# A folded weight product in quarters, four load buffers for the attention steps, and weights loaded in the stage that uses them

## The reference, cut to what matters

```python
def reference(q, k, v, w1, w2, w3, w_out, u1, u2, u3, uo):
    # q, k, v: 8 batches x 8 heads x 576 x 64; D[h][i][j] = gamma_h ** (i - j) for i >= j, else 0
    x = ((q @ k.T) / 8 * D) @ v                    # to 4608 tokens x 512
    x = max(x @ w1, x @ w2, x @ w3) @ w_out        # 512 -> 768 -> 512
    return ((x @ u1) * (x @ u2)) @ u3 @ uo         # 512 -> 1024 -> 1024 -> 512
```

## Time and profile before

| | |
|---|---|
| Time, median of 3 runs | 1333.28 us (1332.85 to 1336.16) |
| The profiled execution | 1333.16 us, of which the span 1331.4 us |
| TensorE busy | 1259.7 us (95%) |
| VectorE, ScalarE, POOL busy | 803.4, 459.7, 452.3 us |
| DMA | 174.37 MB, mean 131 GB/s |

### The profile page before, as it was taken

How to read it: one execution, slowest core, us unless ns; L and a number is a source line. 1 busy time by engine, 2 the same in 40 slices (tenths; PEclk the granted TensorE clock), 3 DMA queues, 4 the chain that set the end, 5 groups by cost and what they waited for, 6 DMA issues and landing times.

```text
span 1331.4 us, 20535 instructions
## 1 busy us (share of the span) xinstructions
PE 1259.7 (95%) x8032; PEld 1235.0 (93%) x8032; DVE 803.4 (60%) x1194; ACT 459.7 (35%) x707; POOL 452.3 (34%) x248
## 2 busy tenths in 40 slices
PE   6999878999999999999999999999999998499999
PEld 5888867999999999999899999999999997499999
DVE  5555668656455555548889677454535537756762
ACT  2112112433333232325455444232323323344442
POOL 2333566602020202006598562202012007635550
PEclk8999988999999999999999999999999999799999
DMA  8778786302020202031655541313313133334441
GB/s 312 235 239 288 252 286 223 133 29 95 25 95 31 89 31 90 31 137 54 224 180 176 174 157 53 109 48 101 104 58 102 52 130 120 130 137 148 155 142 66
DMA packets 82929, 174.37 MB, mean 131 GB/s; under 512 B 8976, under 2 KB 57488, under 8 KB 82832
## 3 DMA queue, kind: packets, MB, share of 16 engines
q1 hardware_dynamic: 82832, 173.05, 37.9%
HBM read 109.58 MB, written 63.44 MB: 130 GB/s over the span
## 4 chain that ended last, share of the span: by engine, by line
PE 74%; DMA 10%; DVE 9%; issue 4%; POOL 1%; SPq 1%; ACT 1%; DVEq 0%; POOLq 0%
PE ps L944 23%; PE ps L945 23%; PE ps L946 23%; DVE clo L699 3%; DMA vks<-vk 3%; DMA u3raw<-u3T 2%; DVE wlo L699 2%; DMA x2d<-h 2%; DMA gd<-h 1%; PE ps L890 1%; PE ps L875 1%; PE ps L900 1%; DVE state L728 1%; DVE probs L709 1%; POOL qdec L499 1%
## 5 line engine op out<-in xcount | busy, mean ns | idle before, releaser
L944 PE MATMUL ps<-chi,whi 128*128 128x384 f32 x2016 | 678.7, 337 | 32.4 <-DVE wlo L699 15.3
L945 PE MATMUL ps<-clo,whi 128*128 128x384 f32 x2016 | 676.4, 336 | 0.0
L946 PE MATMUL ps<-chi,wlo 128*128 128x384 f32 x2016 | 676.3, 335 | 0.0
L499 POOL TENSOR_TENSOR raw<-raw,raw 128x768 f32<-128x768 f32 (+2 forms) x96 | 273.3, 2866 | 536.7 <-DMA raw<-xd 222.0
L944 PEld LDWEIGHTS ps<-chi,whi 128*128 128x128 f32 x2016 | 380.7, 189 | 37.9 <-issue 18.6
L945 PEld LDWEIGHTS ps<-clo,whi 128*128 128x128 f32 x2016 | 380.9, 189 | 0.0
L946 PEld LDWEIGHTS ps<-chi,wlo 128*128 128x128 f32 x2016 | 380.7, 189 | 0.0
L699 DVE TENSOR_TENSOR clo<-raw,chi 128x768 fp32r<-128x768 f32 (+2 forms) x168 | 259.5, 1567 | 16.5 <-ACT chi L622 16.1
L622 ACT CAST chi<-raw 128x768 fp32r<-128x768 f32 (+2 forms) x168 | 180.7, 1081 | 93.8 <-PE ps L946 86.6
L689 ACT COPY w<-ps 128x384 f32<-128x384 f32 x126 | 60.8, 482 | 253.7 <-PE ps L946 252.2
L675 ACT COPY u<-ps 128x384 f32<-128x384 f32 x126 | 60.8, 482 | 168.1 <-PE ps L946 166.6
(11 more groups left out here) (41 smaller groups left out, 917.1 us busy)
## 6 DMA issues: line engine op xcount, KB each, us to landing
qks<-qk SPq DMA_DIRECT2D x32, 576.0 KB, 4.4
vks<-vk SPq DMA_DIRECT2D x32, 576.0 KB, 6.0
gd<-h SPq DMA_DIRECT2D x96, 192.0 KB, 1.9
raw<-gd SPq DMA_DIRECT2D x24, 768.0 KB, 7.2
hd<-h SPq DMA_DIRECT2D x72, 192.0 KB, 1.9
raw<-hd SPq DMA_DIRECT2D x24, 576.0 KB, 5.7
raw<-xd SPq DMA_DIRECT2D x24, 384.0 KB, 5.4
x2d<-h SPq DMA_DIRECT2D x48, 192.0 KB, 2.5
```

Of the source, the lines that this page charges most:

```text
L499: return nc.gpsimd.tensor_tensor(out_, a, b, op)
L944: nc.tensor.matmul(to, w1, x1, start=(start and k == 0), stop=False, skip_group_check=True)
L945: nc.tensor.matmul(to, w1, x2, start=False, stop=False, skip_group_check=True)
L946: last = nc.tensor.matmul(to, w2, x1, start=False, stop=(k == KH[st] - 1), skip_group_check=True)
```

## The change

The 8 blocks of the folded product are cut into quarters (6 matmuls each, over two of the eight slices). Step n does quarter n - 2, for n from 2 to 31, and step 32, which has no scores, does the last two. Loads, casts, splits and copies of `u3`, `uo` and the product follow that rhythm: `u3` block kb is loaded at step 4 kb - 2, cast at 4 kb, split at 4 kb + 1.

`qks` gets 4 buffers instead of 2, `vks` 4 instead of 3, both loaded three steps ahead; `qdec` gets 2. `vks` now lies where positions 4 to 6 of the first token tile are kept, so these are cast and split in the first iterations of stage B, once `valued` is complete. VectorE does a step's splits before `make_state` instead of behind it.

Only weights 0 and 1 and the first tile's raw tokens are loaded in the steps (steps 8, 10 and 12). Weights 2 to 8 are loaded from iteration 0 of stage B on, and each is cast and split in the iteration in which it is summed, one earlier than before.

```diff
 def due(std, ci, io, it, point):
     out = []
-    for tau in range(1, 4 * TILES):
+    for tau in range(4 * TILES):
         table = ci if tau == I * TILES else io if tau == O * TILES else std
-        if it == last_of(tau - 1):
+        if tau and it == last_of(tau - 1):
...
         if it == first_of(tau):
-            out += [(tau, pos) for pos in table.get(("next", point), [])]
+            out += [(tau, pos) for pos in table.get(("next", point), []) if tau or pos > 3]
...
-W_LOAD_AT = {6: 0, 7: 1, 8: 2, 9: 49,
+W_LOAD_AT = {2: 0, 3: 0, 4: 0, 5: 1, 6: 2, 7: 3, 8: 4, 9: 49,
...
-W_SUM_AT = {5: 0, 6: 1, 7: 2, 8: 3, 9: 50,
+W_SUM_AT = {2: 0, 3: 1, 4: 2, 5: 3, 6: 4, 7: 5, 8: 6, 9: 50,
...
-W_SPLIT_AT = {wi: it + 1 for wi, it in W_SUM_AT.items()}
+W_SPLIT_AT = {wi: it + (wi >= FIRST_W[C]) for wi, it in W_SUM_AT.items()}
...
-WC_AT = {3 + 2 * kb: kb for kb in range(FT2)}
 STEPS = NP + 1
-P1_W_LOAD = {12: 0, 14: 1, 19: 2, 20: 3, 21: 4, 23: 5}
...
+WC_FROM = 2
+QUARTERS = 4 * FT2
+def quarters(n):
+    if n == NP:
+        return range(NP - WC_FROM, QUARTERS)
+    return range(n - WC_FROM, n - WC_FROM + 1) if n >= WC_FROM else ()
+U3_LOAD = {max(4 * kb - 2, 0): kb for kb in range(1, FT2)}
+U3_HI = {max(4 * kb, 1): kb for kb in range(FT2)}
+U3_LO = {max(4 * kb + 1, 1): kb for kb in range(FT2)}
+UO_AT = {1: 0, 2: 1, 3: 2, 4: 3}
+WC_READ = {4 * kb + 3 + WC_FROM: kb for kb in range(FT2 - 1)}
+P1_W_LOAD = {8: 0, 10: 1}
+P1_W_SUM = {10: 0, 12: 1}
+P1_RAW = 12
...
         def _(sp):
             def load_qk(n):
-                if n >= 2:
-                    sp.wait_ge(scored, n - 1)
-                    sp.wait_ge(q_decayed, n - 1)
+                if n >= 4:
+                    sp.wait_ge(scored, n - 3)
+                    sp.wait_ge(q_decayed, n - 3)
...
             def load_vk(n):
-                if n >= 3:
-                    sp.wait_ge(valued, n - 2)
+                if n >= 4:
+                    sp.wait_ge(valued, n - 3)
...
-                if 2 <= wi <= 5:
+                if 2 <= wi <= 8:
+                    sp.wait_ge(valued, NP)
                     sp.wait_ge(wc_done, FT2)
+                if wi == 5:
                     for i in range(2):
                         sp.wait_ge(wc_stored[i], 32 * FT2 // 2)
...
             load_qk(0)
             sp.dma_start(dec[:, :, :], decay).then_inc(dec_loaded, 16)
+            load_vk(0)
             sp.dma_start(vtab[:, :, :], vdecay).then_inc(vtab_loaded, 16)
-            load_vk(0)
             sp.dma_start(qtab[:, :, :], qdecay).then_inc(qtab_loaded, 16)
             load_qk(1)
             load_vk(1)
+            load_u3(0)
+            load_uo(0)
+            load_qk(2)
             load_vk(2)
-            load_u3(0)
...
+            load_uo(1)
             for n in range(STEPS):
-                if n + 2 < NP:
-                    load_qk(n + 2)
...
+                if n + 3 < NP:
+                    load_qk(n + 3)
+                if n in U3_LOAD:
+                    load_u3(U3_LOAD[n])
...
+                if n + 3 < NP:
+                    load_vk(n + 3)
                 if n >= 1:
-                    if n + 2 < NP:
-                        load_vk(n + 2)
                     store_x(n - 1)
+                if n - 1 in WC_READ:
+                    store_wc(WC_READ[n - 1])
+            store_wc(FT2 - 1)
...
             def decay_queries(n):
...
-                else:
-                    pool.wait_ge(queried, n)
+                if n >= 2:
+                    pool.wait_ge(queried, n - 1)
...
         def _(act):
             for n in range(STEPS):
+                if n in U3_HI:
+                    split_u3(U3_HI[n])
+                if n in UO_AT:
+                    split_uo(UO_AT[n])
+                if n in WC_READ:
+                    read_wc(WC_READ[n])
                 if n >= 1:
                     read_values(n - 1)
...
+            read_wc(FT2 - 1)
...
         def _(dve):
             for n in range(STEPS):
                 if n < NP:
                     decay_scores(n)
-                    make_state(n)
+                if n in U3_LO:
+                    split_u3(U3_LO[n])
+                if n in UO_AT:
+                    split_uo(UO_AT[n])
...
+                if n < NP:
+                    make_state(n)
...
         def _(pe):
+            def wc_quarter(i):
+                kb, part = divmod(i, 4)
+                if part == 0:
+                    pe.wait_ge(u3_lo, kb + 1)
+                    if kb:
+                        pe.wait_ge(wc_out, kb)
+                if kb == 0:
+                    pe.wait_ge(uo_lo, part + 1)
+                to = ps[:, S_WC, :]
+                for k in (2 * part, 2 * part + 1):
...
             for n in range(STEPS):
                 if n < NP:
                     scores(n)
-                if n in WC_AT:
-                    wc_block(WC_AT[n])
+                for i in quarters(n):
+                    wc_quarter(i)
                 if n >= 1:
                     query_state(n - 1)
```

More of the change, by code:

```diff
@@ L240, in build @@
         wcst = at("wcst", [P, 2, 4, P], f32, o); o += 4096
[L241 to L247, removed]
+        qks = [at(f"qks{i}", [P, KQ_COLS], f32, o + i * KQ_COLS * 4) for i in range(4)]
+        o += 4 * KQ_COLS * 4
+        vks = [at(f"vks{i}", [P, VK_COLS], f32, comb_base[B] + 4 * 6144 + i * VK_COLS * 4) for i in range(4)]
         probs = at("probs", [P, 2, 2, SEQ], f32, o); o += 4 * SEQ * 4
@@ L252, in build @@
         vdec = at("vdec", [P, NC, P], f32, o); o += NC * P * 4
-        qdec = at("qdec", [P, NC, CH], f32, o); o += NC * CH * 4
+        qdec = [at(f"qdec{i}", [P, NC, CH], f32, o + i * NC * CH * 4) for i in range(2)]
+        o += 2 * NC * CH * 4
         state = at("state", [P, NC, P], f32, o); o += NC * P * 4
@@ L459, in _ @@
             for it in range(G + 1):
-                for wi in range(6, NW):
+                for wi in range(2, NW):
                     if W_LOAD_AT.get(wi) == it:
@@ L615, in split_tokens @@
                 if tau == 0:
[L616 to L617 removed]
+                    if pos > 3:
+                        act.wait_ge(valued, NP)
                 elif tau % TILES == 0:
@@ L678, in _ @@
                 splits(it, "p2")
-                for wi in range(5, NW):
+                for wi in range(2, NW):
                     if W_SPLIT_AT.get(wi) == it:
@@ L859, in scores @@
                         keys = SEQ + c * CH
-                        nc.tensor.matmul(ps[:, h, c * CH:(c + 1) * CH], qks[own, n % 2, keys:keys + CH],
-                                         qks[own, n % 2, c * CH:(c + 1) * CH],
+                        nc.tensor.matmul(ps[:, h, c * CH:(c + 1) * CH], qks[n % 4][own, keys:keys + CH],
+                                         qks[n % 4][own, c * CH:(c + 1) * CH],
                                          start=(c == 0), stop=(c == NC - 1), skip_group_check=True)
@@ L864, in scores @@
                     own = slice(h * DH, h * DH + DH)
-                    last = nc.tensor.matmul(ps[:, S_TAIL[h], 0:TAIL], qks[own, n % 2, KQ_COLS - CH:KQ_COLS],
-                                            qks[own, n % 2, SEQ - TAIL:SEQ],
+                    last = nc.tensor.matmul(ps[:, S_TAIL[h], 0:TAIL], qks[n % 4][own, KQ_COLS - CH:KQ_COLS],
+                                            qks[n % 4][own, SEQ - TAIL:SEQ],
                                             start=True, stop=True, skip_group_check=True)
@@ L889, in query_state @@
                     bank, cols = x_cols(c)
-                    last = nc.tensor.matmul(ps[:, bank, cols], state[:, c - 1, :], qdec[:, c - 1, 0:min(CH, SEQ - c * CH)],
+                    last = nc.tensor.matmul(ps[:, bank, cols], state[:, c - 1, :], qdec[n % 2][:, c - 1, 0:min(CH, SEQ - c * CH)],
                                             start=(c == 1 or c == NC), stop=False, skip_group_check=True)
@@ L899, in values @@
                         own = slice(h * DH, h * DH + DH)
-                        last = nc.tensor.matmul(ps[own, bank, cols], vks[n % 3][:, c * P + h * DH:c * P + h * DH + DH],
+                        last = nc.tensor.matmul(ps[own, bank, cols], vks[n % 4][:, c * P + h * DH:c * P + h * DH + DH],
                                                 probs[:, n % 2, h, c * CH:min(SEQ, (c + 1) * CH)],
@@ L903, in values @@
                 last.then_inc(valued, 1)
-            def wc_block(kb):
-                pe.wait_ge(u3_lo, kb + 1)
-                if kb:
-                    pe.wait_ge(wc_out, kb)
-                for k in range(FT2):
-                    if kb == 0 and k % 2 == 0:
-                        pe.wait_ge(uo_lo, k // 2 + 1)
-                    nc.tensor.matmul(ps[:, S_WC, :], u3hi[kb % 2][:, k, :], uohi[:, k, :], start=(k == 0), stop=False)
-                    nc.tensor.matmul(ps[:, S_WC, :], u3hi[kb % 2][:, k, :], uolo[:, k, :], start=False, stop=False)
-                    last = nc.tensor.matmul(ps[:, S_WC, :], u3lo[kb % 2][:, k, :], uohi[:, k, :],
```

(12 more changed lines are left out.)

78 lines of the change are left out of this document (26 added, 52 removed).

## The result

| | before | after |
|---|---|---|
| Median | 1334.72 us (4 runs) | 1297.39 us (4 runs) |
| Ratio after to before | | 0.9718 (95% interval 0.9697 to 0.9739) |
| Profiled execution, its span | 1333.16, 1331.4 | 1297.43, 1295.7 |
| First product of stage B starts at | 235.53 | 197.67 |
| From there to the end of the span | 1095.9 | 1098.0 |

What follows compares the result with a forecast made beforehand. TensorE was taken as the bound, with 51.5 us lost to lateness in the attention stage. Terms: 40.8 - (1.4 - 0.6) - 2.6 - 2 = 35.4 us off 1333.16, so 1298 us, range 1291 to 1311.

Steps and rivals of the forecast that it cites:

- (a): Attention steps: with quarters each takes 5.75 us instead of 9.85 and 4.38 in turn; TensorE's 184.0 us stay.
- (b): Attention loads: issued up to three steps ahead, they cause waits costed at zero after step 2.
- (c): Attention transfers: 1.67 MB per step take 5.0 us at 332 GB/s, under 5.75; cost 0, bound above 10 us.
- (d): Start and attention total: step 2 starts at 17.2, attention ends at 194.7 against 235.53; gain 40.8 us.
- (e): Joint with stage B: TensorE waits 1.4 us for wc_out, and 0.61 us of waiting at the s copy is saved.
- (f): Stage B's first unit: weight 2, loaded only then, delays s(1) and perhaps w(0); loss 2 to 3 us, taken as 2.6.
- (g): VectorE crowded by splits beside POOL: 1 us in stage B's first tile, 1 us in steps 10 to 23.
- the rival in which transfers bind: Attention stage: at 290 GB/s +10, 1308 us, chance 0.08; at 260 GB/s 1330 us, no change, chance 0.02.
- Rival 1: Attention steps: VectorE's splits before make_state make TensorE wait for the state, +10 us, 1308; chance 0.09.

Runs made afterwards that it cites:

- e2_shallow: Changed kernel with queries/keys and values/keys loaded two steps ahead instead of three; 1305.8 us.
- e6_traffic: Changed kernel with one more transfer, 0.59 MB DRAM to DRAM read by nobody, in each of steps 4 to 29; 1298.9 us.
- e1: Changed kernel with its deeper loads, but the folded product in whole blocks in every second step from 5 to 19; 1300.9 us.
- e3: Changed kernel with make_state ahead of the step's splits on VectorE, as before the change; 1317.1 us.
- e4_joint: Changed kernel with ScalarE's last copy of the folded product ahead of its last copy of x; 1297.4 us.
- e8: Changed kernel with whole product blocks and loads two steps ahead together, qdec's second buffer kept; 1305.4 us.
- e5: e4_joint with loads of weights 2, 3 and 4 issued once the folded product is done, ahead of the last stores; 1294.1 us.
- e10_split_early: Changed kernel with make_state ahead of the splits and VectorE's split of a u3 block one step earlier; 1310.2 us.

## Why the prediction was right, and where it was not

- **(a), (b) right in effect.** Steps of 5.77 us (forecast 5.75), no vdec wait after step 2. That the third step of lead is needed only at two places was not seen, nor that POOL's 45.2 us behind the loads say little: in e2_shallow it waited 78.4.
- **(c) wrong in size.** "In a stretch with the engines 0.98 busy they moved 332 GB/s" was taken for their limit. 407 GB/s were moved in e6_traffic with no step longer. TensorE was the bound by a wide margin, not a small one, and the rival in which transfers bind had little in its favour.
- **(d) close.** Step 2 started at 18.00 instead of 17.2, and the last attention matmul ended at 196.3 instead of 194.7, 1.6 us. Half of that is the start: the first step's values decay began 0.4 us later, behind vtab, and step 1 took 5.76 us where it took 5.32 (its first 16 matmuls 2.08 instead of 1.77). The rest is 29 steps at 0.02 us more and a last step 0.2 longer.
- **(e) half right.** The wait was 1.38 (forecast 1.4). The 0.6 us to be saved at the s copy were not: TensorE still waited 0.57 there. ScalarE was idle when the product was done (its copy runs from 199.01 to 199.49, after 1.55 us of idling), so this wait is the copy itself, and was so in the earlier trace rows too.
- **(f) and the clock against each other.** The first unit took 2.44 us more than before (forecast 2.6), but not for the forecast reason alone. The wait for s(1) was 0.73, not 2.6, because TensorE got there later, at half the clock from 200 to 203. Without that, e1 to e3 show it at 1.5, and the first unit still 1.6 us longer than before. So (f) took about 1 us too much, and the granted clock gave it back; the first half's cast fitted before w(0) here, though not in e4_joint, where TensorE came earlier and waited 0.85 us.
- **(g) wrong.** "1 us for them, and 1 us for the same crowding": behind the first unit, stage B kept its distance to the kernel before (counted from its first product, 2.44 us later after unit 0, 2.26 after unit 5, 2.2 at the end), and no attention step was longer for its splits. That VectorE and POOL slow each other down is in the trace (POOL's first sum of weight 2 took 1.50 us beside VectorE's clo, and the four sums of a weight 3.7 to 4.6 us, not the 2.9 of (f)), but on engines with time to spare.
- **The sum was lucky.** The gain on the profiled execution was 35.7 us, the forecast 35.4. In it (d) promised 1.6 us too much and (e) 0.6, and (g) took off 2 us that did not come; the errors cancel.
- **Rival 1** had the danger in the wrong place. I asked what splits ahead of make_state would cost; they cost nothing, and behind it they would have cost 19.7 us.
- **What the sum could not say.** It rested on TensorE's own work being the floor, and in the steps it was right because every cause of lateness was removed at once: TensorE was busy 176.00 of 176 us. It says nothing on which part carried the gain, and its tale of deeper loads and even steps was too simple. By the runs, undoing quarters and depth together costs 8.0 us; on top of that weights 2 to 4 in the steps cost 6.8, late tokens 6.6, and tight due dates of u3 with make_state first 5.3. That is 26.7 of 37.3, if they add, which was not run; quarters and depth did not (3.5 and 8.4 alone, 8.0 together), and the last three sizes are good to a few us only. What is left, some 10 us, was not tried by itself: the rest of the start (step 3 began at 28.24 before, at 26.21 in e8 and at 23.88 after), weight 5, and qdec's second buffer. Whether e5's second and third early weights matter was not tried either.

## What to carry to other kernels

When the bounding engine idles because of work that comes late, forecast from that engine's own work: the floor of TensorE's matmuls gave the end of the attention steps within 1.6 us, while the waits of other engines misled: POOL waited 45.2 us for values/keys in the kernel before, and 78.4 in one that is 29 us faster. On engines that run in order, look for what stands in front of the due work: a split goes where its engine waits anyway, and a load's consumer is issued only when the load has landed. And side work, such as later weights, belongs in steps that are long enough for it, even when it is free by count.

## What the runs showed that I had not expected

- Queues that were busy 0.93 of the time at 319 GB/s moved 407 GB/s over the same 120 us when asked for more, at a share of 1.03: 28% more bytes for 11% more share. In this kernel the busy share of DMA says little on what is left.
- Giving back 1.38 us at the joint gained nothing until weight 2's load, 4.6 us earlier, was moved with it.
- The granted clock fell to 0.50 for 3 us behind waits of 1.38 and 0.57 us in the profiled execution of the kernel after, and not in those of e2_shallow, e3_state_first, e6_traffic and e10_split_early with the same waits.
